# Gram products of a delta-rule recurrence: four banks at the start, an earlier norm computation, three fused steps at the end of an elimination

## What is computed

```
k_n = k / (norm(k) + 1e-6)
for t in range(S):
    y[t]   = q[t] @ state
    v_old  = state^T k_n[t]
    state += beta[t] * outer(k_n[t], v[t] - v_old)
```

## Time and profile before

| | |
|---|---|
| median of 3 runs | 526.88 us (525.96 to 527.99) |
| profiled execution | 527.37 us |
| its span in the trace | 525.5 us |
| busy over the span | PE 87%, DVE 67%, PEld 64%, ACT 59%, POOL 2% |
| records | 17657 |

### The profile page before, as it was taken

The page is one execution under the profiler, slowest core; times in us unless marked ns, Lnnn a source line. Parts: engine busy times, 40 slices in busy tenths (PEclk is TensorE's granted clock), DMA queues, the critical chain, the costliest instruction groups (busy, mean ns, idle before and its releaser), DMA issues.

```text
span 525.5 us, 17657 instructions
## 1 busy us (share of the span) xinstructions
PE 456.1 (87%) x7296; PEld 335.6 (64%) x7296; DVE 353.0 (67%) x1177; ACT 311.8 (59%) x711; POOL 8.2 (2%) x20
## 2 busy tenths in 40 slices
PE   7548877878777788876999599999999999999997
PEld 4434655656555566554433277788888888888885
DVE  3798999999989986422651377656565666556653
ACT  2212788788878888777230356655655655655553
POOL 2000000000000000000000000000000000000000
PEclk9557899999999999989999799999999999999999
DMA  4911344666531233699999600010100100100101
GB/s 168 374 45 41 95 124 143 190 186 186 159 100 34 78 98 111 178 212 230 335 401 412 239 0 1 7 54 1 60 0 0 60 0 0 60 0 0 62 0 61
DMA packets 24295, 59.18 MB, mean 113 GB/s; under 512 B 3104, under 2 KB 11296, under 8 KB 23840
## 3 DMA queue, kind: packets, MB, share of 16 engines
q1 hardware_dynamic: 24224, 58.16, 34.6%
HBM read 53.43 MB, written 4.72 MB: 111 GB/s over the span
## 4 chain that ended last, share of the span: by engine, by line
PE 53%; ACT 20%; DVE 16%; issue 7%; DMA 3%; ACTq 0%; DVEq 0%
PE bank L815 10%; PE bank L817 10%; PE bank L816 10%; ACT zb L827 9%; PE bank L524 6%; ACT nv L870 4%; DVE tmp L1104 4%; DVE tt L1109 4%; PE bank L793 3%; DMA wo<-in_w_out 2%; DVE g_l L1316 2%; DVE g L1313 2%; PE bank L672 2%; ACT state L827 2%; ACT g_h L827 2%
## 5 line engine op out<-in xcount | busy, mean ns | idle before, releaser
L815 PE MATMUL bank<-g_h,wo_h 128*128 128x512 f32 x288 | 113.0, 392 | 2.3 <-DVE g_l L1316 2.1
L1316 DVE TENSOR_TENSOR g_l<-g,g_h 128x512 fp32r<-128x512 f32 x96 | 66.5, 693 | 71.5 <-ACT g_h L827 71.5
L817 PE MATMUL bank<-g_l,wo_h 128*128 128x512 f32 x288 | 112.1, 389 | 0.0
L816 PE MATMUL bank<-g_h,wo_l 128*128 128x512 f32 x288 | 112.1, 389 | 0.0
L827 ACT ACTIVATE g_h<-g 128x512 fp32r<-128x512 f32 x96 | 60.7, 633 | 77.6 <-DVE g L1313 77.6
L1109 DVE TENSOR_TENSOR tt<-tt,tmp 128x110 f32<-128x110 f32 (+35 forms) x366 | 75.1, 246 | 0.2
L1104 DVE TENSOR_TENSOR tmp<-nm,tt 128x110 f32<-128x110 f32 (+35 forms) x366 | 74.8, 245 | 0.2
L1313 DVE TENSOR_TENSOR g<-bank,sig 128x512 f32<-128x512 f32 x96 | 66.2, 689 | 11.2 <-ACT sig L993 6.0
L524 PE MATMUL bank<-zb,kn 128*32 128x192 f32 (+1 forms) x736 | 40.6, 334 | 38.0 <-ACT zb L827 37.5
L827 ACT ACTIVATE zb<-bank 32x192 f32<-32x192 f32 x192 | 61.6, 321 | 6.7 <-PE bank L510 4.6
L815 PEld LDWEIGHTS bank<-g_h,wo_h 128*128 128x128 f32 x288 | 54.0, 188 | 17.5 <-issue 5.7
(11 more groups left out here) (147 smaller groups left out, 448.8 us busy)
## 6 DMA issues: line engine op xcount, KB each, us to landing
kq<-in_kq_t SPq DMA_DIRECT2D x24, 512.0 KB, 4.0
slice<-in_w SPq DMA_DIRECT2D x28, 384.0 KB, 11.2
slice<-in_w SPq DMA_DIRECT2D x12, 512.0 KB, 3.7
slice<-in_w SPq DMA_DIRECT2D x24, 256.0 KB, 5.0
vn<-in_v_nat SPq DMA_DIRECT2D x24, 192.0 KB, 3.1
out_t<-res SPq DMA_DIRECT2D x18, 256.0 KB, 2.0
kn<-in_k_nat SPq DMA_DIRECT2D x23, 192.0 KB, 2.8
win<-in_w_in SPq DMA_DIRECT2D x3, 1024.0 KB, 15.4
```

Source lines behind the costliest of these rows:

```text
L815: eng.matmul(acc[d][:], wo_h[:, f, cols], g_h[:, f % GR], start=(f == 0), stop=False)
L816: eng.matmul(acc[d][:], wo_l[:, f, cols], g_h[:, f % GR], start=False, stop=False)
L817: i = eng.matmul(acc[d][:], wo_h[:, f, cols], g_l[:, f % GR], start=False, stop=(f == NF - 1))
L1316: eng.tensor_tensor(g_l[:, f % GR], g[:, f % GR], g_h[:, f % GR].bitcast(F32), ALU.subtract).then_inc(s_gl, 1)
```

## The change

Four edits. The first four gram products get a bank each, banks 6, 7, 2 and 3, so that none of them waits for a reader; chunk 4 and 5 take banks 6 and 7 again and wait for the first and the second copy and masking; `qs(0)` and `qs(1)` wait until banks 2 and 3 have been read. The matmuls on zeros ahead of them go from five to two. `masked` of chunk 4 moves from before `scales(0)` to after column 0. `nm` is computed right of the diagonal only, as two rectangles, rows 0 to 15 by columns 1 to 31 and rows 16 to 30 by columns 17 to 31. The last two columns (29 and 30) use `scalar_tensor_tensor`, one instruction per row of `tt`: product and sum in one, with the entry of `nm` as a scalar per partition. WARM_AT goes up by one since `scales` now counts one instruction more.

```diff
-WARM_AT = 7 + 4 * 23
+WARM_AT = 8 + 4 * 23
-MASKED_AT = {4: CR + 1, 9: CR + 2, 14: CR + 3, 18: CR + 4, 22: CR + 5}
+MASKED_AT = {0: CR, 4: CR + 1, 9: CR + 2, 14: CR + 3, 18: CR + 4, 22: CR + 5}
...
-        gp = [b[:].rearrange("p (g j) -> p g j", g=NG) for b in bk[6:8]]
+        gp = [b[:].rearrange("p (g j) -> p g j", g=NG) for b in (*bk[6:8], *bk[2:4])]
...
+        def gram_bank(c):
+            return c if c < CR else c % 2
+        def gram_before(c):
+            return c - 1 if c >= CR + 2 else max(c - CR + 1, 0)
...
-                    if c >= 2:
-                        eng.wait_ge(a_gk, c - 1)
-                        eng.wait_ge(v_p, c - 1)
+                    if gram_before(c):
+                        eng.wait_ge(a_gk, gram_before(c))
+                        eng.wait_ge(v_p, gram_before(c))
...
                 if c >= 2:
                     eng.wait_ge(a_y, c - 1)
+                else:
+                    eng.wait_ge(a_gk, c + 3)
+                    eng.wait_ge(v_p, c + 3)
...
-            for _ in range(5):
+            for _ in range(2):
                 eng.matmul(rz[1][:, 0:NG * D], zeros[:, 0:P], zeros[:], start=True, stop=True)
...
-                eng.tensor_tensor(nm[:], gt[:], cneg[:].unsqueeze(1).broadcast_to([P, C, C]), ALU.mult).then_inc(v_c, 1)
+                for rows, cols in ((slice(0, C // 2), slice(1, C)), (slice(C // 2, C - 1), slice(C // 2 + 1, C))):
+                    n, m = rows.stop - rows.start, cols.stop - cols.start
+                    eng.tensor_tensor(nm[:, rows, cols], gt[:, rows, cols], cneg[:, cols].unsqueeze(1).broadcast_to([P, n, m]),
+                                      ALU.mult).then_inc(v_c, 1)
...
+                if j >= C - 3:
+                    for i in range(j + 1, C):
+                        chain.wait(C - 2 - j)
+                        eng.scalar_tensor_tensor(t[:, i, 0:w], t[:, j, 0:w], nm[:, j, i:i + 1], t[:, i, 0:w], ALU.mult,
+                                                 ALU.add).then_inc(v_c, 1)
+                        chain.n += 1
+                    return
...
             masked(CR - 1)
-            masked(CR)
             scales(0)
```

More of the change, by code:

```diff
@@ L472, in gram @@
                     for q in range(HG):
-                        i = eng.matmul(gp[c % 2][quarter(q), 2 * b + a], kq[rows, ring(c), 0, pair_of(b, q)],
+                        i = eng.matmul(gp[gram_bank(c)][quarter(q), 2 * b + a], kq[rows, ring(c), 0, pair_of(b, q)],
                                        kq[rows, ring(c), :, pair_of(b, q)], start=True, stop=True, skip_group_check=True)
@@ L833, in gram_out @@
                     eng.wait_ge(v_t, r - 1)
-                copy(gc[:, r % 2, :, c % CR].rearrange("p j g -> p g j"), gp[c % 2][:, :, 0:C]).then_inc(a_gk, 1)
+                copy(gc[:, r % 2, :, c % CR].rearrange("p j g -> p g j"), gp[gram_bank(c)][:, :, 0:C]).then_inc(a_gk, 1)
             def z_out(c, half):
@@ L1058, in masked @@
                     eng.wait_ge(p_y, c - PR + 1)
-                eng.tensor_tensor(pd[:, ring(c)], gp[c % 2][:, :, C:2 * C], mask[:].unsqueeze(1).broadcast_to([P, NG, C]),
+                eng.tensor_tensor(pd[:, ring(c)], gp[gram_bank(c)][:, :, C:2 * C], mask[:].unsqueeze(1).broadcast_to([P, NG, C]),
                                   ALU.mult).then_inc(v_p, 1)
@@ L1083, in scales @@
                 chain(eng.scalar_tensor_tensor(cneg[:], n2[:], -1.0, cb[:], ALU.mult, ALU.mult))
-                eng.tensor_tensor(nm[:], gt[:], cneg[:].unsqueeze(1).broadcast_to([P, C, C]), ALU.mult).then_inc(v_c, 1)
+                for rows, cols in ((slice(0, C // 2), slice(1, C)), (slice(C // 2, C - 1), slice(C // 2 + 1, C))):
+                    n, m = rows.stop - rows.start, cols.stop - cols.start
+                    eng.tensor_tensor(nm[:, rows, cols], gt[:, rows, cols], cneg[:, cols].unsqueeze(1).broadcast_to([P, n, m]),
+                                      ALU.mult).then_inc(v_c, 1)
                 eng.tensor_copy(tt[r % 2][:].rearrange("p a b -> p (a b)")[:, 0:C * C:C + 1], cneg[:]).then_inc(v_c, 1)
-                chain.n += 2
+                chain.n += 3
                 if r >= 3:
```

## The result

Over 22 runs each, the kernel before took 526.64 us (median, 524.4 to 530.38) and the changed kernel 525.17 us (519.64 to 529.22). The ratio is 0.9958, with a 95% interval of 0.994 to 0.9976: 2.2 us faster, where 5.0 were forecast. 525.17 lies outside the range of 520.0 to 524.6. Three more measurements of the same two kernels gave 0.9957 (0.9932 to 0.9983), 0.9972 (0.9941 to 1.0003) and 0.9926 (0.9905 to 0.9947). In microseconds the four gains are 2.2, 2.3, 1.5 and 3.9, on average 2.5.

A forecast was written before the change was run, and what follows sets the result against it. The prediction took the serial chain up to `solve(0, 0)`, DVE alone from 19.23 us, as the bound. Terms of -4.9 there and -0.1 later gave 522.4 us for the profiled execution, 522.0 for the median, range 520.0 to 524.6.

The forecast's parts named there:

- The sum up to the first solve: Start of `solve(0, 0)`, at 46.25 us before: all front and DVE terms together bring it 4.9 us earlier.
- the overlap of halves: Gram products: a second half runs with the next product's first half, 1.62 us together; four products end at about 11.85.
- the bank each: First four gram products: none waits for a copy or masking, so `squares(0)` starts at 12.5 instead of 14.72, -2.2 us.
- the rival's 3.9: Gram products at full clock: the front gains 3.9 us instead of 2.2, total 520.3 us; chance 0.12.
- `masked(4)`: DVE front: moved after column 0, it frees the reciprocal (-2.5 us), costs 0.34 there and does not wait.
- the fused columns on DVE: Columns 29 and 30: three instructions take 0.6 us instead of six in 1.00, -0.4 us.
- `nm`: Ahead of the first solve: two rectangles take 0.88 us instead of 1.14, -0.26 us.
- the warm-up's end: Before the first solve: PE's warm-up finishes after the inverse, so only 0.27 of the 0.4 us from fusing arrives.
- a microsecond taken from this chain is a microsecond of the total: Chain up to `solve(0, 0)`: nothing else can go on before it, so its saving of 4.9 us counts in full.
- which is as long as before: Loop: its chain has no DVE from chunk 1 on; a length change over 1 us would refute the prediction.
- -0.1 and +-1 for the clock: Loop: later DVE savings are mostly covered, leaving -0.1 us; a clock fall in chunk 0 is open by 1 us either way.
- The front brings nothing: Gram products: halves don't overlap or loads come late, so only -2.7 us remains, total 524.2 us; chance 0.10.

The follow-up runs named there:

- front alone: Kernel before with only a bank each for the first four gram products and two zero matmuls instead of five: ratio 0.9964.
- the pair with the thin load: Changed kernel and kernel before, each loading 16 of 128 partitions of keys and queries for chunks 12 to 23: 520.94 and 525.47 us.
- halved load: Changed kernel with the load of keys and queries in two halves, the second half a chunk later: 0.9992; with 64 idle instructions too, 0.9947.

## Why the prediction was wrong

**The sum up to the first solve held.** -4.4 for -4.9. In the first trace two zero matmuls, the clock at 0.50 for all four products, the overlap of halves and the bank each are right to 0.1 us. That trace records the clock only from 40.65 on, where it goes to 1.00; that it was low before is read from the pace, 7.11 us for four products where two at full clock took 2.44. The rule of the Trainium skill that the throttled clock is the default ("TensorE: Matmul & The Clock Gate", "What's actually happening") was borne out there. It is not so in every execution: in 5 of the 14 traces with two zero matmuls the clock did come up, between 4.7 and 5.9 us, and fell back by 9.3. Even there the gain was not the rival's 3.9 at `squares(0)`, which started at 12.47 to 12.50 (front alone 12.49). Mis-sized were two terms: `masked(4)` (0.37 us of waiting for 0 forecast; the load took longer to land) and the fused columns on DVE (-0.26 for -0.4; three instructions took 0.74), of which the sum had carried only -0.27. `nm` gave 1.14 - 0.90 = -0.24 for -0.26, and the warm-up's end did not bind: DVE released the first solve, not PE.

**The step that failed** is the one that opens the prediction: "a microsecond taken from this chain is a microsecond of the total", with its companion, a loop "which is as long as before". The sum gave the loop -0.1 and +-1 for the clock. In the traces the loop took 195.8 and 196.1 us before, and 198.1, 201.5, 194.5 and 201.0 in the changed kernel, 2.8 more on average, while the first solve came 4.4 and 4.1 us earlier in the first two pairs. What the traces show in place of an unchanged loop: packets of 16 KB on an instruction queue share the DMA engines with the loads, and behind one that comes late PE stands still in the midst of a product. Where that happens moved with the number of instructions that PE has ahead of the loop, of which the change took 12 away. I priced the three matmuls by their duration alone.

How far this is shown: that the burst of the `kq` load takes the missing time is shown by the pair with the thin load, 4.5 us apart, against 2.5 on average with the full one, and by the two loops, then of one length. That the stalls' place goes with the layout of the instruction stream is shown by the traces: 4 records to go in chunk 1 in six of the seven traces that have the changed kernel's stream or the front's, the thin and the halved load among them, and 13 in chunk 10 in all six that have that of the kernel before without idle instructions. That the layout also decides how much time is lost is supported, not shown. The kernels whose stream stands as before have 0.9925 to 0.9939, the changed kernel 0.9926 to 0.9972, and these overlap. The link in between, that PE waits for the instruction packet and the packet for the load, rests on the order of events: of 62 stalls over 0.4 us in the loops of the 20 traces, 60 end 2.2 to 2.9 us behind the start of a packet of that queue, and packets are some 4.6 us apart. There is no experiment that moves the packet alone. How much of a stall's price is the lower clock behind it stays open.

The chain of waits does not name it: a stall of this kind appears there as "issue", and the kernel before had 1 us of it at 136 us, which I passed over as one of many.

**The rivals.** None of them was this one. "The front brings nothing" gave the nearest time, 524.2, but by luck: at the first solve the front did bring its part, and the loop took it back.

## What to carry to other kernels

Look for a stall on "issue" in the middle of a group of like instructions, 2 to 3 us behind a packet of the instruction queue, and look where the big loads lie beside it. Here such stalls took up to 2.13 us each, more than half of the edits of this change are worth. A gain measured after adding or removing instructions on the engine that stalls may contain a change of layout too. Here some 2 of 4.5 us did not arrive, and leaving out most of one load brought them back. Measure a small change more than once, beside the kernel that it is compared with, and with some idle instructions added, before believing or rejecting it: the changed kernel's four measurements alone run from 1.5 to 3.9 us.

## What the runs showed of the hardware that was not expected

- An instruction queue moved 54 packets of 16 KB in this kernel, in the loop one every 3.4 to 8.4 us. At the stalls over 1 us shown above, but for the one at 239.13, the packet moved only as a 512 KB load was ending, and PE went on 2.2 to 2.9 us after the packet's start. The Trainium skill ("Runtime: NRT & Kernel Launch", "Instruction fetch mechanics") says that instructions come in blocks of 16 KiB, which the packets confirm, and that the cost of crossing from one to the next is mostly hidden. For most packets the traces agree: none has more than 10 stalls over 0.4 us at its some 40 packets of the loop. At single crossings they don't: 1.20, 1.95, 2.05 and 2.13 us.
- A wait for a semaphore that is long there is not free on PE: 64 such instructions in one block kept PE idle for 6.12 us ahead of the first `ks`, some 0.1 us each (an estimate, 6.12 / 64). In the changed kernel the first solve then came at 43.54, against 41.30 to 41.81 without them; 4 blocks of 16 in idle stretches left it at 41.56. In the kernel before it stayed at 46.17, since the warm-up behind the block took 4.73 us and not 6.52.
